# Two attention scores and two mixture layers on one core: inputs in longer runs, guard columns, a new order of the work

## The reference

```
factor = 4; Sd = S // factor; scale = 1 / sqrt(D)
q_d, k_d, v_d = means of q, k, v over groups of 4 tokens       # 144 tokens each
out_up  = repeat(softmax(scale * q_d k_d^T) v_d, 4)            # "down" attention
scores  = where(|i - j| < 4, scale * q k^T, -1e9)              # "local" attention: 7 keys a token
x       = out_up + softmax(scores) v                            # both softmaxes divide by (sum + 1e-9)
h = x @ w_in1;  P = a0 + a1 h + a2 h^2 + a3 h^3
Q = 1 + |b0| |h| + |b1| h^2;  x = (P / (Q + 1e-6)) @ w_out1
h = x @ w_in2;  out = (h * tanh(log(1 + exp(min(h, 20))))) @ w_out2
```

## Time and profile before

| | before |
|---|---|
| median of three runs | 479.26 us |
| profiled execution, time | 478.56 us |
| its span, first to last instruction | 476.4 us |
| TensorE busy | 461.9 us |
| VectorE, ScalarE, GpSimd busy | 398.1, 306.2, 214.9 us |
| mean granted TensorE clock | 0.985 of full |
| moved by DMA | 29.71 MB in 46436 packets, 31792 of them under 512 bytes |

### The profile page before, as it was taken

How to read it: one execution, slowest core, us unless ns; L and a number is a source line. 1 busy time by engine, 2 the same in 40 slices (tenths; PEclk the granted TensorE clock), 3 DMA queues, 4 the chain that set the end, 5 groups by cost and what they waited for, 6 DMA issues and landing times.

```text
span 476.4 us, 11017 instructions
## 1 busy us (share of the span) xinstructions
PE 461.9 (97%) x4318; PEld 338.3 (71%) x4318; DVE 398.1 (84%) x671; ACT 306.2 (64%) x565; POOL 214.9 (45%) x224
## 2 busy tenths in 40 slices
PE   6999799999999999999999999999999999999996
PEld 5667689898889788899998976444444555557662
DVE  7787799999787887878878788998899888878894
ACT  4477578888566585678877776566545555554542
POOL 5789935579352422117422635762625122212122
PEclk8997899999999999999999999999999999999999
DMA  5989733610801100020200221132000200000101
GB/s 120 247 202 296 159 92 90 161 24 2 190 1 37 24 3 3 1 89 1 89 4 1 89 89 45 45 90 88 0 1 0 90 0 2 0 1 1 66 3 44
DMA packets 46436, 29.71 MB, mean 62 GB/s; under 512 B 31792, under 2 KB 39984, under 8 KB 46384
## 3 DMA queue, kind: packets, MB, share of 16 engines
q1 hardware_dynamic: 45168, 28.71, 22.3%
q10 hardware_dynamic: 1216, 0.30, 0.3%
HBM read 26.64 MB, written 2.36 MB: 61 GB/s over the span
## 4 chain that ended last, share of the span: by engine, by line
PE 77%; POOL 11%; DVE 4%; ACT 3%; issue 3%; DMA 1%; SPq 0%; ACTq 0%; POOLq 0%
PE bank L602 33%; PE bank L643 18%; PE bank L623 17%; PE bank L565 3%; POOL g_l L1061 2%; POOL w L1049 2%; PE bank L509 1%; POOL work L1047 1%; DMA late<-in_k 1%; POOL late L1013 1%; POOL late L1037 1%; POOL late L1049 1%; PE bank L552 1%; ACT late L684 1%; POOL raw L1047 1%
## 5 line engine op out<-in xcount | busy, mean ns | idle before, releaser
L1061 POOL TENSOR_TENSOR g_l<-work,g_h 128x512 f16<-128x512 f32 (+2 forms) x81 | 90.4, 1116 | 212.0 <-ACT g_h L769 179.1
L602 PE MATMUL bank<-x_h,w 128*128 128x256 f16 (+1 forms) x640 | 102.5, 264 | 2.7 <-DVE work L929 2.7
L623 PE MATMUL bank<-g_h,w 128*128 128x256 f16 (+1 forms) x640 | 101.3, 262 | 0.5 <-POOL g_l L1061 0.4
L602 PE MATMUL bank<-x_h,late 128*128 128x512 f16 (+2 forms) x384 | 96.9, 326 | 0.0
L759 ACT ACTIVATE bank<-work,coef 128x512 f32<-128x512 f32 (+2 forms) x81 | 52.3, 646 | 64.3 <-DVE work L925 63.1
L643 PE MATMUL bank<-late,g_h 128*128 128x512 f16 x288 | 92.1, 379 | 0.1
L602 PE MATMUL bank<-x_l,w 128*128 128x256 f16 (+1 forms) x320 | 84.6, 264 | 0.0
L623 PE MATMUL bank<-g_l,w 128*128 128x256 f16 (+1 forms) x320 | 83.8, 262 | 0.0
L602 PEld LDWEIGHTS bank<-x_h,w 128*128 128x128 f16 x640 | 61.4, 99 | 8.5 <-DVE work L929 2.9
L623 PEld LDWEIGHTS bank<-g_h,w 128*128 128x128 f16 x640 | 60.8, 98 | 8.1 <-issue 2.1
L602 PE MATMUL bank<-x_l,late 128*128 128x512 f16 (+2 forms) x192 | 62.6, 326 | 0.0
(11 more groups left out here) (103 smaller groups left out, 804.9 us busy)
## 6 DMA issues: line engine op xcount, KB each, us to landing
raw<-in_moe_w_in SPq DMA_DIRECT2D x10, 512.0 KB, 5.6
raw<-in_moe_w_out SPq DMA_DIRECT2D x10, 512.0 KB, 4.3
late<-in_k SPq DMA_DIRECT2D x16, 144.0 KB, 4.1
late<-in_v SPq DMA_DIRECT2D x8, 288.0 KB
late<-in_v SPq DMA_DIRECT2D x32, 72.0 KB
out<-w SPq DMA_DIRECT2D x9, 256.0 KB, 2.3
late<-in_moe_w_in SPq DMA_DIRECT2D x4, 512.0 KB, 3.6
late<-in_moe_w_out SPq DMA_DIRECT2D x4, 512.0 KB, 4.5
```

What stands on the lines that cost most here:

```text
L602: last = pe.matmul(ps, w_in(l, wp)[:, kk, at], x[:, kk, t0:t0 + n], start=(kk == 0 and wp == 0 and x is x_h), stop=(kk == KD - 1 and wp == 1))
L623: last = pe.matmul(ps, w_out(0, wp)[:, f, 128 * d:128 * (d + 1)], g[q % 4][:, i * n:(i + 1) * n], start=False, stop=(f == FT - 1 and d % 2 ...
L1061: pool.tensor_tensor(g_l[q % 4][:, 0:w], num[q % 4][:, 0:w], g_h[q % 4][:, 0:w], ALU.subtract).then_inc(g_rest, 1)
```

## The change

- A step is now 256 or 320 tokens (eight or ten blocks of 32) in place of twice 288, so the first step is the first block of the first layer.
- q of step 0 and k of the first two pairs (p < FAST = 2) come in one transfer each, with runs of four (q) or eight rows (k), 1 and 2 KB. Later ones keep runs of 256 bytes, with 64 partitions for q and 72 for k. The tokens lie across partitions in another order, so put_q and put_k write with a step of 4 or 5 or of 8 elements, and pool_k reads its bank with a step of 72. The fast k pairs take four banks and 16 transposes each in place of two and 6, with a ScalarE copy and a VectorE reduce per bank; fast q takes 16 transposes and four copies.
- Windows of v are one transfer a head of 39 rows at a stride of 32 rows, out of one flat view of v, and one more transfer where they would pass either end of the array.
- The coefficients a and b are loaded by ScalarE, behind q.
- The 1e-9 of a softmax's sum is a constant guard column beside the probabilities, which the reduce includes; the addition of it goes.
- The mask contains the borders of a batch; the two edge matmuls a step go. GpSimd builds one group of 38 columns, copies it, and sets four borders.
- The memsets of both window tiles shrink to three rows.
- y of block 3 (of 0 to 4) lies in banks 6 and 7, that of the others in 4 and 5.
- In the last tile VectorE takes output row 7 out when its own matmuls are done; ScalarE stores row 8 itself. (Rows are of 128 tokens.)
- All ticks, fillers and TWO_BANKS are new.

The core of the diff:

```diff
-    TP = 96
-    TR = S // TP
     HEADS = 4
     SD = S // FACTOR
     QT = 32
     KW = QT + 2 * (FACTOR - 1)
     PAD = FACTOR - 1
     HALF = S // 2
-    U = HALF // QT
+    PARTS = (256, S - 256)
+    MOST = max(PARTS)
...
-    TWO_BANKS = 36.5538
+    TWO_BANKS = -41.6157
-    FILLER = {"out_local": 1, "turn_k": 8, "score_local": 6, "turn_p_end": 24, "turn_q": 3, "turn_p": 4, "turn_d": 3, "out_down": 10}
-    FIRST_FILLER = 1
+    FILLER = {"turn_k": 10, "turn_p": 12, "score_down": 2, "out_local": 6, "turn_p_end": 19}
+    FIRST_FILLER = 0
...
+    FAST = 2
+
+    def jobs(name, s):
+
+        return 4 if name == "turn_k" and s < FAST else JOBS.get(name, 0)
...
+        APART = len(BLOCKS1) - 2
+        y_bank = [banks[6:8] if b == APART else banks[4:6] for b in range(len(BLOCKS1))]
...
+        p_loc_sum = [x.rearrange("p u (h c) -> p (u h) c", h=2)[:, :, 0:KW + 1] for x in p_loc]
+        p_dwn_sum = [carve(HEADS * (SD + 1)).rearrange("p (g c) -> p g c", g=HEADS) for _ in range(2)]
+        p_dwn = [x[:, :, 0:SD] for x in p_dwn_sum]
...
+                if p < FAST:
+                    sp.dma_start(k_raw[p % 2][0:NP, :].rearrange("p (h n) -> p h n", h=2),
+                                 k[bb, hp:hp + 2].rearrange("h (p r) d -> p h (r d)", r=R)).then_inc(k_loaded[p % 2], 16)
+                    return
                 for hh in range(2):
-                    sp.dma_start(k_raw[p % 2][0:TP, :, D * hh:D * (hh + 1)],
-                                 k[bb, hp + hh].rearrange("(r p) d -> p r d", p=TP)).then_inc(k_loaded[p % 2], 16)
+                    sp.dma_start(k_raw[p % 2][0:NP, :].rearrange("p (r n) -> p r n", r=R)[:, :, D * hh:D * (hh + 1)],
+                                 k[bb, hp + hh].rearrange("(p r) d -> p r d", r=R)).then_inc(k_loaded[p % 2], 16)
...
+                    begin = (H * bb + 2 * pair + h) * S + t0 - PAD
+                    dst = v_win[s % 2][HP * (h % 2):HP * (h % 2) + WR, h // 2, :, :]
+                    if begin < 0:
+                        sp.dma_start(dst[PAD:WR, 0:1, :], rows_of(0, WR - PAD, 1)).then_inc(win_loaded[s % 2], 16)
+                        lo = 1
+                    elif begin + QT * (hi - 1) + WR > B * H * S:
+                        hi -= 1
+                        last = begin + QT * hi
+                        sp.dma_start(dst[0:B * H * S - last, hi:hi + 1, :],
+                                     rows_of(last, B * H * S - last, 1)).then_inc(win_loaded[s % 2], 16)
+                    sp.dma_start(dst[:, lo:hi, :], rows_of(begin + QT * lo, WR, hi - lo)).then_inc(win_loaded[s % 2], 16)
...
+                for job in range(jobs("turn_k", p)):
+                    ps, hh, j = open_job(("turn_k", p, job)), job // 2, job % 2
+                    for i in range(FACTOR):
+                        r = FACTOR * j + i
+                        own = D * (R * hh + r - hh) if p < FAST else 2 * D * r
+                        last = pe.transpose(ps[:, NP * i:NP * (i + 1)], k_raw[p % 2][0:NP, own:own + 2 * D], ident[0:NP, 0:NP])
...
-                        if t == (U - 1) * half:
-                            border = slice(KW - PAD, KW) if half else slice(0, PAD)
-                            pe.matmul(to[:, :, border], ident_b[0:QT, 0:QT],
-                                      edge[:, :].rearrange("p (h n) -> p h n", h=2), start=False, stop=False)
...
+                    if b == APART:
+                        wait_emptied(pe, holder[6 + k])
+                    elif b > 0:
+                        held = b - 1 if b < APART else b - 2
+                        pe.wait_ge(y_rest, 2 * held + k + 1)
                     else:
                         pe.wait_ge(consts, 4)
-                    pe.matmul(y_bank[k][:, :], zeros[:, 0:128], zeros[:, :], start=True, stop=False)
+                    pe.matmul(y_bank[b][k][:, :], zeros[:, 0:128], zeros[:, :], start=True, stop=False)
...
+                        if q == NT - 1 and row == ROWS - 2:
+                            last.then_inc(row_whole, 1)
...
+                    to = q_t[s % 2][:, i, 0:n].rearrange("c (p r) -> c r p", p=TQ)
+                    ps = banks[bank_of[("turn_q", s, i)]]
+                    for own, at in ((slice(0, 64), 0), (slice(64, 128), n)) if s == 0 else ((slice(0, 128), 0),):
+                        ins = act.activation(to[own, :, :], ps[own, at:at + n].rearrange("c (r p) -> c r p", p=TQ),
+                                             ACT.Copy, scale=D ** -0.5)
+                    ins.then_inc(act_emptied, 1)
...
+                        to = k_bd[p % PAIRS][own, hh, PAD:PAD + S].rearrange("c (p r) -> c r p", r=R)
+                        ins = act.activation(to[:, FACTOR * j:FACTOR * (j + 1), :],
+                                             ps[own, 0:HALF].rearrange("c (r p) -> c r p", r=FACTOR), ACT.Copy, scale=1.0)
...
+                    if b == len(BLOCKS2) - 1:
+                        row = ROWS - 1
+                        wait_row(act, row)
+                        act.dma_start(out[128 * row:128 * ROWS, :], rows[:, DM * row:DM * ROWS]).then_inc(out_stored, 16)
...
+            act.dma_start(q_raw[0][0:TQ, 0:HEADS * D * tokens(0) // TQ].rearrange("p (h n) -> p h n", h=HEADS),
+                          q[0, 0:HEADS, 0:tokens(0)].rearrange("h (p r) d -> p h (r d)", p=TQ)).then_inc(q_loaded[0], 16)
+            act.dma_start(a_raw, a.rearrange("(o n) -> o n", o=1).to_broadcast([128, 4])).then_inc(coef_loaded, 16)
+            act.dma_start(b_raw, b.rearrange("(o n) -> o n", o=1).to_broadcast([128, 2])).then_inc(coef_loaded, 16)
...
+                for n in range(jobs("turn_k", p)):
+                    job, j = ("turn_k", p, n), n % 2
                     wait_emptied(dve, job, by="act")
-                    ps = banks[bank_of[job]][:, 0:HALF].rearrange("c (t i) -> c t i", i=FACTOR)
-                    dve.tensor_reduce(kd_t[p % PAIRS][:, NP * j:NP * (j + 1)], ps, AX.X, ALU.add).then_inc(dve_emptied, 1)
+                    own = slice(64 * (n // 2), 64 * (n // 2) + 64) if p < FAST else slice(0, 128)
+                    ps = banks[bank_of[job]][own, 0:HALF].rearrange("c (i t) -> c t i", i=FACTOR)
+                    to = kd_t[p % PAIRS][own, :].rearrange("c (t j) -> c j t", j=2)
+                    dve.tensor_reduce(to[:, j, :], ps, AX.X, ALU.add).then_inc(dve_emptied, 1)
...
-                link(dve.tensor_scalar(total, total, 1e-9, None, ALU.add))
...
+            dve.memset(v_win[0][0:PAD, 0, 0, :], 0.0).then_inc(zeroed, 1)
             for i in range(2):
-                dve.memset(v_win[i][0:WP, :, :, :], 0.0).then_inc(zeroed, 1)
-                dve.memset(p_loc[i][:, :, KW:HP], 0.0).then_inc(zeroed, 1)
+                dve.memset(p_loc[i][:, :, KW + 1:HP], 0.0).then_inc(zeroed, 1)
+                dve.memset(p_loc_sum[i][:, :, KW:KW + 1], 1e-9).then_inc(zeroed, 1)
+                dve.memset(p_dwn_sum[i][:, :, SD:SD + 1], 1e-9).then_inc(zeroed, 1)
...
+            pool.tensor_copy(masks[:, 1:, :], masks[:, 0:1, :].to_broadcast([128, more, KW])).then_inc(mask_step, 1)
...
+            for half in range(2):
+                U = PARTS[half] // QT
+                for i in range(2):
+                    c = U * i + (U - 1) * half
+                    border = slice(KW - PAD, KW) if half else slice(0, PAD)
+                    row, col = 32 * (c % 4), 2 * (c // 4)
+                    pool.memset(mask[half][row:row + QT, col:col + 2, border], NEG).then_inc(mask_step, 1)
```

373 lines of the change are left out of this document (199 added, 174 removed), and 8 rows, old and new, of the table STAGES.

## The result

The changed kernel took 488.03 us in the median of 4 runs (484.96 to 494.18), the kernel before 479.04 in the same session (478.66 to 479.39). The ratio is 1.0166, 95% interval [1.0117, 1.0216]: slower by 1.7%, 8.0 us, where 471.4 was forecast.

The account below looks back on a forecast made before the run. TensorE, busy 97% of the span, was taken to bound the kernel. Terms 1 and 2 together -5.3, then -1.2, -1.0 and -0.4 gave -7.9 us: span 468.5, median 471.4, range 466.5 to 477.5.

Parts of the forecast that it names:

- Unknown costs: Strided q and k copies, pooled reduces, load spread: 0 to 2.3 us for 26 writes before hidden 0; 0.4 taken.
- Rival B: ACT's strided writes are dear: at +0.8 each ACT is 12 us late at hidden 0, time 483.5; chance 0.10.
- Term 1: Start of the layers: hidden tile 0 at 44.5 us in place of 47.8, ends 40 to 48.
- sum (a): PE's queue before hidden 0: fewer fillers and edges, more transposes, no wait for k; 47.8 comes down to 44.1.
- Term 2: Hidden 0 to first output tile: 17 us in place of 19.0, bounds 15.8 and 21; first output at 61.5.
- rival A: POOL at slowed rates replaces the stall ahead of the first g_l: first output 65.5, time 475.4; chance 0.13.
- Term 3: PE work of the rest: turn_p 3 done ahead, edge matmuls gone, transposes smaller but more; -1.2 us.
- Term 4: y in two more banks: PE's waits of 0.24 and 0.75 at blocks 3 and 4 go; -1.0 us.
- Term 5: The end: DVE's row released three matmuls earlier, ACT stores the last row itself; -0.4 us.
- C: Prologue comes down to PE's queue: hidden 0 at 40 and 17 behind it, time 466.9; chance 0.10.
- D: Loads of k and windows crowd some DMA engines: 3 us, 474.4 if all reaches hidden 0; chance 0.05.
- E: New orders win nothing, terms 3 to 5 alone hold: time 476.7; chance 0.07.

Follow-up runs that it names:

- e2: Changed kernel with ScalarE's q and k copies reading PSUM at a stride and writing q in a row, k in runs of four; 478.82 us, ratio 0.9983.
- e1: Changed kernel with q and k copies and k's pooled reduce over bytes in a row, output not the reference's; 478.86 us, ratio 1.0001.
- e7: e2 with coefficients used behind the prologue, k0 issued first and SP waiting for k0 and k1 before v; 476.26 us, ratio 0.9949.
- e9: Changed kernel with four mends: those of e7 plus the second layer's order of before (e5); 476.29 us, ratio 0.9946.
- e11: e9 with each head's window of v in three transfers, as before, in place of one; 476.56 us, ratio 0.9945.
- e13: e9 with POOL's norm_local 2 ahead of its rest of unit 1; 476.92 us, ratio 0.9965.
- e12: e8 with coefficients used behind the prologue and issued by SP behind k0 and k1; 470.59 us, ratio 0.9831.
- e17: e9 with unit 1's weights finished by DVE in place of POOL; 474.62 us, ratio 0.9921.
- e16: e8 without the two extra banks for y; 476.12 us, ratio 0.9935.
- e8: Kernel before plus only mask borders, guard columns, two banks for block 3's y and the last row's store; 474.70 us, ratio 0.9917.
- e10: e9 with the first k pairs in 256-byte runs, two transfers each, as before; 478.09 us, ratio 0.9982.
- e4: Changed kernel with the first k pair's load issued ahead of the second and v in SyncE's queue; 487.55 us, ratio 1.0155.
- e5: e2 with the second layer's weight units (16 to 31) in the order of before; 476.66 us, ratio 0.9958.
- e15: e8 with coefficients used behind the prologue, still issued by SP ahead of k0; 474.13 us, ratio 0.9892.
- e18: e12 with unit 3's weights finished by DVE in place of POOL; 471.83 us, ratio 0.9875.

## Why the prediction was wrong

**Unknown costs.** This is the step that failed most. 0.4 us was put down for 26 writes before hidden 0, and nothing behind it; the runs show 8.8 us for 50 writes (changed kernel against e2). Two things were wrong. The reach: 24 of the writes stand behind hidden 0, and they had no term. The size: I took +0.18 a write as the far end, from POOL's adds over every fourth element, and took none of it; it was 0.29 for k and 0.30 for q (against e1). POOL reads such a row, ACT writes it, and e2 shows that the two sides have different prices. The rule of the Trainium skill cited there (SBUF — State Buffer, "Door 1: The DMA port swizzle") pointed to this and the trace agrees in the direction: a copy of 64x288 took 0.41 us in a row and 0.69 at 32 bytes from element to element.

**Rival B** was the right mechanism and was dismissed at the wrong point. It added ACT's busy time up to hidden 0 and found that ACT alone could bear up to 0.65 a write. That holds only if each copy may wait for its turn. But each stands in a chain from turn over copy to score and reduce, and DVE waited 12.2 us for ACT's k copies in all, where it had waited 2.0 before and waits 5.5 in e2. So more than half of each added us came through (8.8 of 14.5), though before hidden 0, where PE had looked 88% busy, only 1.5 of it came (49.87 against 48.38): 3.5 came between hidden 0 and the first block and 4.1 behind it, where the prediction had looked for nothing. B's own number, 483.5, asked for 0.8 a write. The chance of 0.10 rested on a slack that no row had shown.

**Term 1.** Forecast 44.5, after 49.87. It comes out only in e7 and e9 (43.6, 43.3) and in e11 and e13 (43.7, 44.9), which are built on e9. It had the wait for k gone since 20 fillers and turn_q stand ahead of it; k0 as third in SP's queue landed at 9.5, and the coefficients behind q held ACT until 9.44. I had named the coefficient loads as being ACT's and had priced that as nothing. The order of the first issues is worth 2.0 us there (e7) and 2.9 on the other base (e12). That hidden 0 at 43.3 then agrees with sum (a), 44.1, is in part luck: the sum kept before's stretches at half clock (0.89 on average), and e9's profile has none (1.00).

**Term 2** was mis-sized by 6 us: 17 to the first output, 23 in e9 with nothing else wrong. The prediction asked the right question ("late next is POOL itself") and had POOL through the two rests, with norm_local 2 next, by some 42: 27.8 us of work at the unslowed durations from 7 us on, and 7 of waits. In e9 norm_local 2 starts at 47.82. Stage 7 to 47.82 of e9:

```profile
7.00:47.82 40.82, 36.82 (x570) 29.92 (x568) 32.64 (x68) 27.69 (x58) 31.80 (x37) 1.00 0.97 229
```

So it is 31.8 us of work, 4.0 more than counted, and 9.0 of waits, 2.0 more. The rests that I had at 3.55 took 4.6 and 5.8, and this although I cited the slowed rows beside it and gave them to rival A. Rival A's time for it, 475.4, is close to e9's 476.3; its mechanism, POOL in the stall's place, is what e13 and e17 show. Another part of the 23 is the half clock behind the wait: 0.85 over the stretch, 3.4 us of full speed.

**Term 3** has two errors of opposite sign. The new second layer's order cost 1.6 us, which no step looked at: I took "the rest" as only losing PE work and never sorted the ticks of units 16 to 31 against g_l. In its place the rest stretch of e9 is 2.3 us under before, where terms 3 and 4 had 2.2 together. Edges and guard columns give 2.25 in e16, against 0.8 forecast for the edges alone; the sums' lost step, costed at nothing, is in it, in the stretch where DVE was full (the two aren't parted). Turning p of step 3 ahead and the smaller transposes then give nothing that is to be seen: e9's rest is 0.6 longer than e8's.

**Term 4** was 1.0, measured 0.65 in e8 against e16: the waits went, and 0.76 of them came back at POOL's g_l a little later. With the new order of the second layer (changed kernel, e2, e7) that wait isn't there. **Term 5**: from the start of the last matmul to the span's end are 3.59 us, before 4.22, 0.6 less where 0.4 was forecast.

**Rivals C, D, E.** C asked for POOL to be on time and fell with term 2. D's crowding isn't there for windows (e11); for the first k's no run parts it from the rest (e10). Its neighbour, one of the first loads holding up another, is real (e4, e7). E's 476.7 lies near e5's and e9's numbers for other reasons.

**The sum.** The forecast ratio was 0.9836, measured 1.0166: 15.8 us apart. The mends, one upon the other, take the changed kernel down to 0.9921 (e17): 8.8 by the read stride, 1.6 by the coefficients' later use and the first loads (e7 against e2), 0.1 by the second layer's order, though its trace shows 1.6, and 1.2 by POOL's relief. That is 11.7. Some 4 us stay open. They lie ahead of the first block, which was forecast at 61.0 (0.5 ahead of the first output) and which every kernel with the new loads reached at 65.4 or later, wherever its hidden 0 lay; waits for loads, POOL and stretches at half clock hide one another there, and no run of mine parts them.

## What to carry to other kernels

Price a new access pattern by side (read, write) and engine, and when no row has it, give its upper end to every instruction on a tight chain; when a layout change forces a stride, put it on the PSUM read of the copy, which gave back all that it had cost here (e2 is as fast as e1). An engine's busy sum shows what it can bear only if its work can wait; ask who stands behind each instruction. Look for a clock below 1 in short pieces of a stretch: a mean of 1.00 over 400 us hid 1.7 us. The order of the first few DMA issues, two small ones included, moved this kernel by 2 to 3 us, where all the small parts together gave 4.

## What was not expected of the hardware

- ACT copying 64x288 fp32 from PSUM: 0.406 us in a row (e1), 0.472 with a stride of 288 bytes on the read and runs of 16 bytes on the write (e2), 0.693 with a stride of 32 bytes on the SBUF write (changed). Its copies of q, 256 to 320 a partition: 0.397 in a row, 0.396 with a stride of 256 bytes on the read, 0.696 with 16 to 20 bytes on the write. DVE's reduce of k read PSUM at a stride of 288 bytes in 0.458 and in a row in 0.452 (e1), medians over 64 and 128 partitions.
- Two loads of 4 and 2 values broadcast to 128 partitions, issued ahead of the first k, put ACT's first k copy 2.5 us later (8.09 in e15 against 5.62 in e12; 8.12 in e8 against 6.48 in e18), though they delay its issue by 0.9. Issued behind q they landed at 9.4 themselves (changed).
- POOL's TENSOR_SCALAR over 128x512 took 0.62 us at 42.04 in e9, and 1.59 at 44.19, where DVE was in its own rests (43.30 to 46.85); two v adds took 1.52 or 2.40.
- The mean clock before hidden 0 was 0.83 in the changed kernel's profile and 1.00 in e9's. e9 ran at 2.4 GHz into its wait of 3.55 us; PE was idle from 46.1, the clock fell to 1.2 GHz at about 48.3 while it was, and rose again at about 55, with PE busy since 49.7 (0.50 between).
